# Rounds 0 to 4 of a chunked linear-attention scan: other PSUM banks, another engine for one product, another order

## What is computed

```python
for t in range(S):
    kt, vt, rt, wt = (k[:, :, t], v[:, :, t], r[:, :, t], w[:, :, t])
    cur = np.einsum('bhd,bhe->bhde', u[None] * kt, vt)
    y[:, :, t] = np.einsum('bhd,bhde->bhe', rt, state + cur)
    state = wt[:, :, :, None] * state + np.einsum('bhd,bhe->bhde', kt, vt)
...
x = _moe_ref(x=x, **moe_kwargs)
return _moe2_ref(x=x, **moe2_kwargs)
```

## Time and profile before

| | |
|---|---|
| time, median of 3 runs | 405.87 us (405.72 to 406.1) |
| the profiled execution's own time | 405.78 us |
| its span in the trace | 404.3 us |
| TensorE busy | 392.1 us, 97% of the span |
| VectorE, GpSimd, ScalarE busy | 188.4, 161.6, 114.3 us |
| share of the chain that ended last | PE 90%, DVE 5%, issue 2%, POOL 1%, ACT 1% |

### The profile page before, as it was taken

The page is one execution under the profiler, slowest core; times in us unless marked ns, Lnnn a source line. Parts: engine busy times, 40 slices in busy tenths (PEclk is TensorE's granted clock), DMA queues, the critical chain, the costliest instruction groups (busy, mean ns, idle before and its releaser), DMA issues.

```text
span 404.3 us, 6836 instructions
## 1 busy us (share of the span) xinstructions
PE 392.1 (97%) x2638; PEld 377.0 (93%) x2638; DVE 188.4 (47%) x397; ACT 114.3 (28%) x224; POOL 161.6 (40%) x180
## 2 busy tenths in 40 slices
PE   5999899999999999999999999999999999999997
PEld 4788788898899999899999999999999999999996
DVE  5889988678664452314443736350132123103301
ACT  3257526565412020673001212340021012002200
POOL 5764787684425662585899970000000000000000
PEclk9999999999999999999999999999999999999999
DMA  9999598553110202002113310000100100000001
GB/s 146 129 234 227 97 207 198 118 99 92 46 41 2 78 2 78 2 1 79 39 49 109 117 42 0 2 0 21 39 2 0 41 20 2 19 21 19 2 19 39
DMA packets 60129, 25.03 MB, mean 62 GB/s; under 512 B 51136, under 2 KB 58176, under 8 KB 60096
## 3 DMA queue, kind: packets, MB, share of 16 engines
q1 hardware_dynamic: 60096, 24.58, 27.8%
HBM read 22.22 MB, written 2.36 MB: 61 GB/s over the span
## 4 chain that ended last, share of the span: by engine, by line
PE 90%; DVE 5%; issue 2%; POOL 1%; ACT 1%; DVEq 0%; POOLq 0%; ACTq 0%
PE bank L1062 25%; PE bank L1064 24%; PE bank L1063 24%; PE bank L1152 4%; PE bank L1076 3%; PE bank L1148 3%; DVE suf L846 2%; PE bank L1187 2%; PE bank L1113 2%; PE bank L1205 1%; PE bank L1120 1%; PE bank L1131 1%; DVE pre L858 1%; POOL rp L555 1%; DVE am L882 1%
## 5 line engine op out<-in xcount | busy, mean ns | idle before, releaser
L754 ACT ACTIVATE ha_hi<-bank 128x384 fp32r<-128x384 f32 x48 | 23.6, 492 | 113.1 <-PE bank L1064 113.1
L989 DVE SCALAR_TENSOR_TENSOR ha_lo<-bank,ha_hi 128x384 fp32r<-128x384 f32 x48 | 26.8, 558 | 50.2 <-ACT ha_hi L754 50.2
L1062 PE MATMUL bank<-c_hi,ha_lo 128*128 128x384 f32 x144 | 48.2, 335 | 0.0
L1064 PE MATMUL bank<-c_hi,ha_hi 128*128 128x384 f32 x144 | 48.1, 334 | 0.0
L1064 PE MATMUL bank<-u2T_hi,c_hi 128*128 128x384 f32 x144 | 48.1, 334 | 0.0
L1063 PE MATMUL bank<-c_lo,ha_hi 128*128 128x384 f32 x144 | 48.1, 334 | 0.0
L1062 PE MATMUL bank<-u2T_hi,c_lo 128*128 128x384 f32 x144 | 48.1, 334 | 0.0
L1063 PE MATMUL bank<-u2T_lo,c_hi 128*128 128x384 f32 x144 | 48.1, 334 | 0.0
L994 DVE TENSOR_TENSOR x<-bank,x 128x384 f32<-128x384 f32 x12 | 6.7, 558 | 65.3 <-PE bank L1064 65.3
L1062 PE MATMUL bank<-sg_hi,z_lo 128*128 128x384 f32 x96 | 32.5, 338 | 0.0
L1064 PE MATMUL bank<-sg_hi,z_hi 128*128 128x384 f32 x96 | 32.1, 334 | 0.0
(11 more groups left out here) (142 smaller groups left out, 886.2 us busy)
## 6 DMA issues: line engine op xcount, KB each, us to landing
raw<-in_moe_w_ch SPq DMA_DIRECT2D x12, 384.0 KB, 3.1
kc<-in_k SPq DMA_DIRECT2D x12, 192.0 KB, 4.4
rc<-in_r SPq DMA_DIRECT2D x12, 192.0 KB, 5.0
vn<-in_v SPq DMA_DIRECT2D x12, 192.0 KB, 5.0
raw<-in_moe_w_sg SPq DMA_DIRECT2D x6, 384.0 KB, 4.0
out<-x SPq DMA_DIRECT2D x12, 192.0 KB, 1.9
raw<-in_moe_w_in SPq DMA_DIRECT2D x4, 384.0 KB, 4.8
raw<-in_moe_w_tok SPq DMA_DIRECT2D x4, 384.0 KB, 3.3
```

The costliest lines, as they stand in the source:

```text
L754: sc.activation(ha[0][:, i, :], bank[:, 0:HALF], ACT.Relu).then_inc(act_out, 1)
L989: ve.scalar_tensor_tensor(ha[1][:, i, :], bank[:, 0:HALF], 0.0, ha[0][:, i, :].bitcast(F32), ALU.max, ALU.subtract).then_inc(dve_out, 1)
L1062: te.matmul(dst, left[1], right[0], start=first, stop=False)
L1064: return te.matmul(dst, left[0], right[0], start=False, stop=last)
```

## The change

In rounds 0 to 4:

- **Banks.** The decays of odd chunks up to 5 go to bank 6 (`decay_bank`), so `turn_w(n + 2)` waits for `forward(n)` and no longer for `forward(n + 1)`. The state products of rounds 0 to 4 go to bank 7 (`state_bank`), so bank 1 serves k alone.
- **`scale_k` on GpSimd** for chunks 0 to 5: ScalarE copies k of bank 1 to a new tile `kt` (`take_kt`), GpSimd multiplies it by `suf`. In exchange r of chunk 0 alone is scaled by VectorE, straight from bank 2 (`scale_first_r`).
- **Orders.** TensorE: `turn_w(n + 2)` right behind `turn_k(n + 1)`, `state_products(n)` ahead of `outputs(n)`. VectorE: `state(n)` and `backward(n + 2)` ahead of `y_tile(n)`, `mark_range` behind `state(4)`. GpSimd: `diagonal_v`, `rk_products`, `scale_k`, `scale_r`, `rku_products` (the two halves of `diagonal_products` part). ScalarE: `take_state(n - 1)` in round n, range passes 2 and 3, 4 to 6, 7 and 8, and 9 in rounds 1 to 4 (before: 7 to 9 in round 3).
- **Loads.** Another order; `check_w` in two halves; k, r, v of chunks 5, 5 and 4 and w of 6 ahead of the first raw weights.

In all rounds: `turn_kp` and `take_k` are left out in rounds 5 and 11, whose `kn` nobody reads. From round 5 on the order is the old one but for GpSimd: both `split_low` of `w_in` 2 and 3 and `scale_r(6)` come ahead of `diagonal_v(5)`. The four filler matmuls of round 0 go; three more stand ahead of round 0 instead.

```diff
-        bw, b1, b2, bs, by, bc = ps[0], ps[1], ps[2], ps[3:5], ps[5], ps[7]
+        b1, b2, bs, by = ps[1], ps[2], ps[3:5], ps[5]
+        bc = ps[7][:, 4 * PART - CHECKS:4 * PART]
+        def decay_bank(n):
+            return ps[6] if n <= YR and n % 2 else ps[0]
+        def state_bank(n):
+            return ps[7] if n < YR else b1
...
             load_w(2)
-            load_v(1)
             load_k(2)
             load_r(2)
+            load_v(1)
             load_w(3)
+            load_w(4)
+            load_v(2)
             load_k(3)
             load_r(3)
-            load_v(2)
-            load_w(4)
             load_w(5)
-            sp.dma_start(check_w[:, :].rearrange("p (h x) -> p h x", h=H),
-                         w[1].rearrange("h (p j) d -> p h (j d)", j=PJ)).then_inc(check_in, 16)
+            load_check(0)
             load_k(4)
             load_r(4)
             load_v(3)
+            load_check(1)
+            load_k(5)
+            load_r(5)
+            load_v(4)
+            load_w(6)
             load_raw(0)
             load_raw(1)
...
+            def scale_k(n):
+                pool.wait_ge(kt_copied, n + 1)
+                pool.wait_ge(suf_done, NP * (n + 1))
+                if n:
+                    pool.wait_ge(qk_done, n)
+                    pool.wait_ge(kn_turned, states(n - 1))
+                gp.tensor_tensor(kp[0:QP, :, :], kt[0:QP, :, :], suf[0:QP, n % 2, :, 1:PART + 1], ALU.mult
+                                 ).then_inc(kp_done, 1)
...
                 split_low("w_in", 2)
+                split_low("w_in", 3)
                 for n in range(YR, NCH):
+                    if n == YR:
+                        scale_r(n + 1)
                     chunk(n)
                     chunk_end(n)
...
+            scale_k(0)
+            rk_products(0)
+            rku_products(0)
+            for n in range(YR):
+                diagonal_v(n)
+                rk_products(n + 1)
+                scale_k(n + 1)
+                scale_r(n + 1)
+                rku_products(n + 1)
             pool.wait_ge(ok_counted, 1)
...
+            def take_kt(n):
+                act.wait_ge(kt_done, n + 1)
+                if n:
+                    act.wait_ge(kp_done, n)
+                sc.copy(kt[0:QP, :, :], pairs(b1)[0:QP, :, :]).then_inc(kt_copied, 1)
...
-            checks = {1: (2, 3), 2: (4, 5, 6), 3: (7, 8, 9)}
+            checks = {1: (2, 3), 2: (4, 5, 6), 3: (7, 8), 4: (9,)}
             for n in range(NCH):
-                take_k(n)
+                if n % NC < NC - 1:
+                    take_k(n)
+                if n < YR:
+                    take_kt(n + 1)
+                if 1 <= n <= YR:
+                    take_state(n - 1)
...
-            scale_k(0)
+            scale_first_r()
             backward(1)
-            for n in range(NCH):
+            for n in range(YR):
                 mask(n, 0)
                 mask(n, 1)
+                if n == 0:
+                    diagonal(0)
+                forward(n + 1)
+                if n:
+                    backward(n + 2)
+                state(n)
+                if n == 0:
+                    backward(2)
                 if n == YR - 1:
                     mark_range()
-                if n == 0:
-                    diagonal(0)
+                y_tile(n)
+                if n == YR - 1:
+                    count_range()
+                diagonal(n + 1)
+            bound_x()
...
-            keep_busy(1)
+            keep_busy(4)
             for n in range(NCH):
                 scores(n)
-                turn_kp(n)
+                if n % NC < NC - 1:
+                    turn_kp(n)
                 if n + 1 < NCH:
                     turn_k(n + 1)
+                if 0 < n < YR:
+                    turn_w(n + 2)
                 for job in slot_jobs(n, 0):
                     product(*job)
                 if n + 1 < NCH:
                     turn_r(n + 1)
-                if n == 0:
-                    keep_busy(2)
+                if n < YR:
+                    state_products(n)
                 outputs(n)
```

More of the change, by code:

```diff
@@ L201, in build @@
     suf = put("suf", [PART, 2, NP, PART + 1])
+    kt = put("kt", [PART, NP, PART])
     cursor[0] = GT
@@ L225, in build @@
         raw_in = [sem(f"raw_in{i}") for i in range(SLOTS)]
-        check_in = sem("check_in")
+        check_in = [sem(f"check_in{i}") for i in range(2)]
         ub_in, gln_in, bsg_in = sem("ub_in"), sem("gln_in"), sem("bsg_in")
@@ L360, in load_v, with load_check @@
                 sp.dma_start(vn[:, n % VR, :].rearrange("p (h d) -> p h d", h=H), rows(v, n)).then_inc(v_in[n % VR], 16)
+            def load_check(i):
+                half = RAW // 2
+                sp.dma_start(check_w[:, half * i:half * i + half].rearrange("p (h x) -> p h x", h=H // 2),
+                             w[1, H // 2 * i:H // 2 * i + H // 2].rearrange("h (p j) d -> p h (j d)", j=PJ)
+                             ).then_inc(check_in[i], 16)
             def load_raw(n):
@@ L399, in _ @@
             for n in range(3, NCH):
[L400 to L406, removed]
+                if n > 3:
+                    if n + 2 < NCH:
+                        load_k(n + 2)
+                        load_r(n + 2)
+                    if n + 1 < NCH:
+                        load_v(n + 1)
+                    if n + 3 < NCH:
+                        load_w(n + 3)
                 for i in later.get(n, []):
@@ L676, in take_k @@
             def take_k(n):
-                act.wait_ge(kn_turned, n + 1)
-                if n and n % NC:
+                act.wait_ge(kn_turned, states(n))
+                if n:
                     act.wait_ge(ds_done, states(n - 1))
@@ L810, in _ @@
                     take_job(*job)
-                if n % NC < NC - 1:
+                if n >= YR and n % NC < NC - 1:
                     take_state(n)
@@ L1100, in turn_r @@
                 if n:
-                    pe.wait_ge(kn_copied, n)
+                    pe.wait_ge(kn_copied, states(n - 1))
+                    if n == 1:
+                        pe.wait_ge(rp_done, 1)
+                    else:
+                        pe.wait_ge(rt_copied, n - 1)
                 turn(b2, rc[:, n % KR, :, :]).then_inc(rt_done, 1)
@@ L1116, in turn_kp @@
             def turn_kp(n):
-                pe.wait_ge(rt_copied, n + 1)
+                if n == 0:
+                    pe.wait_ge(rp_done, 1)
+                else:
+                    pe.wait_ge(rt_copied, n)
                 for p in range(NP):
@@ L1125, in state_products @@
                 wait_ring(pe, v_in, n)
-                pe.wait_ge(kn_copied, n + 1)
-                pe.wait_ge(kp_done, n + 2)
+                pe.wait_ge(kn_copied, states(n))
+                if n >= YR:
+                    pe.wait_ge(kp_done, n + 2)
+                elif n:
+                    pe.wait_ge(st_done, n)
                 for p in range(NP):
@@ L1158, in sum_range @@
                 pe.wait_ge(ok_marked, 1)
-                te.matmul(bc[:, 0:CHECKS], ones[:, :], okf[:, :], start=True, stop=True).then_inc(ok_summed, 1)
+                te.matmul(bc, ones[:, :], okf[:, :], start=True, stop=True).then_inc(ok_summed, 1)
             def free_bank(job):
@@ L1246, in keep_busy @@
                 for _ in range(m):
-                    te.matmul(ps[6][:, 0:PART], ident[:, :], ident[:, :], start=True, stop=True)
+                    te.matmul(ps[7][:, 0:PART], ident[:, :], ident[:, :], start=True, stop=True)
             pe.wait_ge(consts, CONSTS)
```

70 lines of the change are left out of this document (37 added, 33 removed).

## The result

The changed kernel takes **403.63 us** (median of 5 runs, 401.82 to 404.56) against 405.87 (405.72 to 406.1): a ratio of 0.9943, 95% interval 0.9915 to 0.997. It is faster, since the interval leaves out 1, but by 2.24 us, half of the 4.5 that 401.4 would have been; the median lies inside the range (400.2 to 403.8), by 0.17 us, and two of the five runs lie above it. The runs lie far apart: 401.82, 404.3, 403.63, 403.52 and 404.56 us, at mean granted clocks of 1.0, 0.996, 0.995, 0.995 and 0.992. The run at clock 1.0 is the profiled one, so the rows of after show the kernel without what cost the other four their 1.7 to 2.7 us. One run of the kernel before, taken beside later kernels, is a slow one (488.76 us at 0.757) and stands in no number here.

A forecast was written before the change was run, and what follows sets the result against it. The prediction took waits among engines to bound the first rounds and full TensorE the stretch from 110 us; 4.0 us by round 6 plus 0.44 in round 11, off 405.78, gave 401.4 us, range 400.2 to 403.8.

The forecast's parts named there:

- The start: Ahead of round 0: VectorE scales r directly, so the scores come at 9.4, 0.86 before the 10.28.
- Round 1's link: From scores of round 0 to those of round 1: GpSimd's products, not TensorE, set it at 7.5 us; round 1 begins at 16.9.
- Rounds 1 to 3: TensorE is the longest engine at 6.3 us a round against 7.29; three rounds bring the scores of round 4 to 35.8.
- Round 4: TensorE's `sum_range` waits for VectorE's `mark_range`, 6.9 us from the scores: 0.66 lost, 0.2 for the product; round 5 at 42.95.
- Round 5: Takes 9.7 us against 10.60, with a new wait of 0.35 for the flag; round 6 begins at 52.6, 4.0 earlier.
- that cover: Round 5: TensorE's mixing product and round 6 scores hide `yt(5)` coming some 2 us late; cost nothing, without it 403.4.
- GpSimd's `kp`: The product `kp` moved to GpSimd in the first rounds takes 1.24 us, as `rp` does; bounds 0.67 and 1.35.
- the rival that made GpSimd the bound: `scale_k` in rounds 0 to 5 holds up `rp`, for which scores wait; `kp` at 3.0 us gives 409.4; chance 0.05.
- the loss behind round 6: VectorE or a GpSimd split is late in rounds 6 to 9 by TensorE's gain; 405.9, no change; chance 0.04.
- Loads: Rival: w of chunk 6 lands no earlier than 39.7, stopping `turn_w(6)` 1.9 us; 402.7, at worst about 404.4; chance 0.11.
- the ring: First rounds: TensorE, ScalarE and VectorE wait on each other in a circle; second decay bank frees `turn_w`, second state bank `turn_k`.
- the clock: Rival: TensorE's 2.2 us idle before round 1's scores brings slow matmuls back, costing at most 2.6 us, 404.0; chance 0.04.

## Why the prediction was right, and where not

**The sign and the path were right, the size was not.** In the execution without a fall the time is 401.82, 0.42 over the forecast, and all of that stands by the scores of round 6 (53.02 against 52.6). That it comes so close is in part luck: the start came 0.8 late and rounds 1 to 3 took 0.33 more, the link, round 4 and round 5 took 0.7 less. By the steps of the prediction:

- *The start*: forecast 9.4, came at 10.20, 0.8 late. The step that failed is "the filler matmuls of round 0 stood in idle time: nothing". The change did not only take them out of round 0, it put more of them ahead of it, and these ran up to the scores, 0.84 behind `rp`. With one filler there the scores came at 9.52, but between 9.71 and 10.32 in the profiles of the other kernels that have one: how long the first matmuls stay slow counts as well.
- *Round 1's link*: 7.35 against 7.5. GpSimd's products set it, as forecast; with one product fewer it took 6.82. TensorE stood idle for 1.41 of it, where 2.2 were forecast.
- *Rounds 1 to 3*: 6.41 each against 6.3, 0.33 in all. It lies in the state products and outputs (in round 1 from 20.49 to 23.96, 3.47 us, against 0.6 + 2.61 + 0.1).
- *Round 4*: 6.99 against 7.15; the wait for the range count is there. The prediction's terms for VectorE add up to 6.84, not 6.9; `mark_range` ended 6.62 behind the scores.
- *Round 5*: 9.25 against 9.65. The flag stands at 44.94 (44.8 forecast), but TensorE does not wait for it, where 0.35 of waiting was forecast. `y_tile(5)` waits until 50.81 (50.8 forecast) while TensorE does not wait for it: that cover held.
- *GpSimd's `kp`*: 1.19 against 1.24; the rival that made GpSimd the bound is refuted, and so is the loss behind round 6 (the scores of round 6 are 3.61 earlier, the end 3.96).
- *Loads*: the rival is refuted. w 6 landed 4.0 us after its issue at 31.4, and `turn_w(6)` came at 38.75; with the old order nothing moved in the rounds either.

**Two reasons inside the right sum were wrong, and a third was worth less than it seems.** The claim that the second state bank takes `turn_k` out of the ring is worth nothing, once k is copied out early and the state stands ahead of `y_tile`: with one bank the rounds are the same 6.41. And scaling k on GpSimd does not shorten rounds 1 to 3: on VectorE they took 6.35. It costs 0.59 in the link and saves 0.82 in round 4 and 0.19 in round 5; up to round 6 that is a gain of about 0.25. The second decay bank, with the place between `turn_k` and `turn_r` that it gives `turn_w`, made 1.36 of the 2.5 us that rounds 1 to 3 gained; the kernel without it lost 2.8, but 1.2 of that to another order on VectorE. For the other 1.1 us of these rounds the new orders are left, and no run tried them by themselves.

**The term that was missing from the time is the clock.** It stood among the rivals at a chance of 0.04, as a stretch behind the idle time of round 0. The sign that the prediction named for it, matmuls of round 1 at the length of the first ones, is in the second profile of the changed kernel (1.06). It was priced at up to 2.6 us, and the stretch in round 1 cost 1.54; its chance was far too low. The windows that it quotes for a clock of 1.00 begin at 8 us, behind those first transposes; windows over the transposes read 1.00 too. The median of 403.63 is 1.8 above the execution without a fall.

What the runs show of it is this. On one chip, 10 of 12 runs with an open link fell (the changed kernel again, no fillers; idle for 1.41 and 1.56 us in the profiles), and none of 8 with fillers in it. With the first five runs of the changed kernel it is 14 of 17. So fillers in the link all but stop the falls; that is shown. With fillers in the link and the stall at the range count either as in after or gone (five kernels), 1 of 23 fell. With the stall lengthened to an idle 1.07, 4 of 5; with it filled or removed, 0 of 14. Two profiles show the granted clock at 0.50 right behind that stall, so it is likely that it can bring a fall as well. But the kernels with it filled or removed ran on another chip than the one with it lengthened; that the fillers and not the chip made the difference is not shown. The argument against this rival, "the gap is short beside the 7.5 us of the whole link", is what failed. The Trainium skill (TensorE: Matmul & The Clock Gate, HAM oscillation) has the gate that takes TensorE back to half rate when it idles between bursts, and these runs agree so far: 0.50 soon after an idle 1.41, where the page's own example has longer waits.

Three things stay open. Only profiled executions show where a fall lies, and the one without any filler fell behind the stall of round 4 and not behind its open link, though that stall is the same in kernels whose runs hardly fell; how the link bears on a fall 26 us later was not tried. The length of an idle stretch alone does not decide: with one decay bank TensorE stood 1.01 for the flag, and none of five runs fell. And the kernel before has 0.70 idle in rounds 2 to 4 and fell in none of the runs compared; what sets its waits apart from the 0.19 shown ahead of `sum_range` in after wasn't tried.

## What to carry to other kernels

When a change shortens a wait on TensorE's rounds, look at the idle stretches that it opens at the first and the last of them: a link idle for 1.4 us, with its fillers moved away, cost here 1.8 of 4 us in the median, and nothing in the execution that was profiled, so read the mean granted clock of every run beside the times. Put fillers into the stretch that they are to cover, behind the last instruction before it, and not ahead of work that is about to become ready; shorten the stretch itself where an order on another engine can. And test the parts one by one, and read in which round each shows: of two added banks and one moved product, one bank gave about half of what the rounds gained, the other bank none.

## What was not expected of the hardware

- The fall is not the same in each execution of one program: of eleven runs of the changed kernel three stayed at 1.0, seven show the mean of one stretch, one that of two. The three stretches that profiles caught, one each in three kernels, cost about 1.5 us in their rounds (1.54, 1.49, 1.47).
- TensorE's first matmuls do not come down to their later length at the same time in each execution: a turn of four at 8.90 still took 1.06 with the old order of the loads, and one at 8.14 took 0.60 with the new one. The granted clock reads 1.00 in all windows there, from 3 to 11 us in both traces, so the difference shows only in the matmuls' own times. With one filler ahead of them, the scores of round 0 came at 9.52 in one trace and at 10.32 in another.
